# A fused attention and expert kernel: f32 weighted values replaced by three rounded passes, the row of maxima copied by DMA, weight splits moved into the first block

## The reference

```python
q_bits = (np.einsum('bhsd,dk->bhsk', q, proj) > 0).astype(np.int64)
k_bits = (np.einsum('bhsd,dk->bhsk', k, proj) > 0).astype(np.int64)
mask = q_bucket[:, :, :, None] == k_bucket[:, :, None, :]
scores = np.where(mask, scale * np.matmul(q, k.transpose(0, 1, 3, 2)), -1000000000.0)
attn = np.exp(scores - np.max(scores, axis=-1, keepdims=True))
attn = attn / (np.sum(attn, axis=-1, keepdims=True) + 1e-09)
x = np.matmul(attn, v)                      # heads side by side: 1536 x 512
h = x @ w_in                                # 512 x 2048
g = np.where(h > 0.0, h, np.exp(np.minimum(h, 0.0)) - 1.0)
x = g @ w_out                               # 2048 x 512
# rows with x @ w_skip > 0 get x + gate * (relu(x @ w1[e]) @ w2[e]), e = argmax(x @ w_gate)
```

## Time and profile before

| | us |
|---|---|
| median of three runs | 715.51 |
| the profiled execution: time | 718.39 |
| the profiled execution: span from first to last instruction | 716.5 |
| PE busy (matmuls) | 678.6 (95%) |
| DVE, ACT, POOL busy | 326.7, 238.2, 192.9 |

### The profile page before, as it was taken

How to read it: one execution, slowest core, us unless ns; L and a number is a source line. 1 busy time by engine, 2 the same in 40 slices (tenths; PEclk the granted TensorE clock), 3 DMA queues, 4 the chain that set the end, 5 groups by cost and what they waited for, 6 DMA issues and landing times.

```text
span 716.5 us, 9192 instructions
## 1 busy us (share of the span) xinstructions
PE 678.6 (95%) x3472; PEld 574.7 (80%) x3472; DVE 326.7 (46%) x475; ACT 238.2 (33%) x365; POOL 192.9 (27%) x179
## 2 busy tenths in 40 slices
PE   4999999998999999999999999999998975999996
PEld 3677767676777777799999989989997954989995
DVE  6766656565666654133232223222314257446542
ACT  1233334333333334333342334233422321334330
POOL 3322253535162430659120002000002034112111
PEclk9999999999999999999999999999999995999999
DMA  7456656564555530412020002000366765699200
GB/s 176 118 129 141 165 125 163 125 162 96 139 117 133 116 89 10 131 44 67 1 90 1 1 0 88 0 0 0 146 200 206 241 238 188 237 346 334 89 11 24
DMA packets 69235, 83.95 MB, mean 117 GB/s; under 512 B 35540, under 2 KB 45780, under 8 KB 69200
## 3 DMA queue, kind: packets, MB, share of 16 engines
q1 hardware_dynamic: 67920, 79.83, 38.1%
q0 software_dynamic: 1280, 3.65, 1.6%
HBM read 56.64 MB, written 8.44 MB: 91 GB/s over the span
## 4 chain that ended last, share of the span: by engine, by line
PE 85%; DMA 5%; DVE 4%; SPq 2%; ACT 1%; issue 1%; POOL 0%; POOLq 0%; DVEq 0%; ACTq 0%
PE banks L1179 18%; PE banks L1166 18%; PE banks L1125 15%; PE banks L1290 8%; PE banks L1305 6%; PE banks L1093 5%; DMA k_hi_lo_T<-qk_lo_T 4%; PE banks L1112 4%; PE banks L1113 4%; SPq L312 2%; PE banks L1077 2%; PE banks L1197 1%; DVE g_lo L839 1%; PE banks L1101 1%; DVE row_max L770 1%
## 5 line engine op out<-in xcount | busy, mean ns | idle before, releaser
L1125 PE MATMUL banks<-probs,v_ones 128*128 128x384 f32 x384 | 152.8, 490 | 0.3 <-ACT o_and_den L629 0.3
L1166 PE MATMUL banks<-x_hi,w_split 128*128 (+1 forms) x512 | 142.4, 339 | 0.8 <-DVE g L860 0.8
L1179 PE MATMUL banks<-w_split,g_hi 128*128 128x512 f32 x384 | 122.2, 399 | 4.8 <-DVE g_lo L839 4.8
L860 DVE SCALAR_TENSOR_TENSOR g<-exp_min_h,banks 128x384 f32<-128x384 f32 x64 | 35.5, 554 | 198.0 <-ACT exp_min_h L672 197.8
L645 ACT ACTIVATE probs<-banks 128x768 f32<-128x768 f32 x96 | 77.8, 811 | 132.3 <-PE banks L1113 132.3
L770 DVE TENSOR_REDUCE row_max<-banks 128x1 f32<-128x768 f32 x96 | 91.4, 957 | 66.5 <-PE banks L1093 64.7
L1166 PEld LDWEIGHTS banks<-x_hi,w_split 128*128 128x128 f32 x512 | 94.2, 189 | 4.0 <-DVE g L860 1.1
L669 ACT ACTIVATE exp_min_h<-banks 128x384 f32<-128x384 f32 x64 | 31.5, 492 | 181.5 <-PE banks L1166 181.5
L1166 PE MATMUL banks<-x_lo,w_split 128*128 (+1 forms) x256 | 86.3, 337 | 0.0
L1179 PEld LDWEIGHTS banks<-w_split,g_hi 128*128 128x128 f32 x384 | 71.3, 190 | 18.0 <-DVE g_lo L839 6.0
L1093 PE MATMUL banks<-k_hi_rows_T,q_hi_rows_T 96*128 96x384 f32 x192 | 76.8, 487 | 7.8 <-DMA k_hi_lo_T<-qk_lo_T 7.5
(11 more groups left out here) (155 smaller groups left out, 835.0 us busy)
## 6 DMA issues: line engine op xcount, KB each, us to landing
expert_w<-in_moe_w SPq DMA_DIRECT2D x32, 1024.0 KB, 5.3
w_raw<-in_moe_w_in SPq DMA_DIRECT2D x16, 256.0 KB, 3.5
w_raw<-in_moe_w_out SPq DMA_DIRECT2D x16, 256.0 KB, 3.7
qk_nat<-in_q SPq DMA_DIRECT2D x16, 192.0 KB, 4.1
qk_nat<-in_k SPq DMA_DIRECT2D x16, 192.0 KB, 4.3
v_nat<-in_v SPq DMA_DIRECT2D x16, 192.0 KB, 3.0
q_hi_rows_T<-qk_hi_T SPq DMA_DIRECT2D x16, 192.0 KB, 2.7
k_hi_rows_T<-qk_hi_T SPq DMA_DIRECT2D x16, 192.0 KB, 3.0
```

The source lines that it names most:

```text
L860: dve.scalar_tensor_tensor(gb[:, j % 2, :], e_neg[:, j % 2, :], -1.0, banks[:, j % 2, 0:BN], ALU.add, ALU.max).then_inc(s_["g_ready"], 1)
L1125: mm = pe.matmul(banks[:, 6 + b, 0:HALF], v_ones[h % 2][:, s, :], probs[:, n % 4, b * HALF:b * HALF + HALF], start=(s == 0), stop=(s == QT ...
L1166: mm = pe.matmul(banks[:, j % 2, 0:BN], w, x, start=(c == 0 and w is hi and x is x_hi), stop=(c == KC - 1 and w is lo))
L1179: mm = pe.matmul(banks[:, 2 + t, :], g, W[:, j, part, :], start=(j == 0 and i == 0), stop=(j == FT - 1 and i == 2))
```

## The change

- `weighted` makes three passes in float32r (high by high, low by high, high by low; L1211 to L1213 of the changed kernel) in place of one f32 matmul, and follows its step by four steps in place of two. `p_hi` is made by ACT (`high_probs`), `p_lo` by DVE for the steps 1 and 2 of a head and by POOL for the other four (`low_probs`). V is split by ACT (`high_of_v`) and POOL (`low_of_v`); nothing of V's mean is left, so `VSUM`, `mean_of_v`, `centre_v` and the addition in `normalise` go.
- Two extra columns of ones in `p_hi` give the sum that the 1e-9 of the denominator needs; ACT adds it in `outputs`.
- The maxima are one row: DVE writes six partitions of 128 and a DMA on SP brings them to the query row (`copy_minus_maxima`), between the copies of the high rows and of the low rows.
- `T`, `MAX_T` and `BITS` stand earlier or later in the steps; SP's other loads stand ahead of the row copies.
- Four weights are split in attention, at every second head, and twelve in the first block, by ACT (`high_of_w`) and DVE (`low_of_w`). The last three weighted units stand in the first block. x is split in smaller pieces.
- Expert 0's weight is split by POOL in pieces of 512 columns, its second half behind the first gather.

```diff
-EARLY = 9
+EARLY = 4
+LAG = 4
+RING = 4
+WIDE = HALF + 2
+ON_DVE = (1, 2)
...
     a, b = h + 1, h + 2
-    plan = [[], [("MAX", a, 0), ("MAX", a, 1)], [("MAX", a, 2), ("MAX", a, 3)],
-            [("MAX", a, 4), ("MAX", a, 5), ("T", b, 0)], [("VSUM", b, 0), ("MAX_T", a, 0)], [("BITS", b, 0)]][s]
+    plan = [[[], [("MAX", a, 0)], [("MAX", a, 1)]], [[], [("MAX", a, 2)], [("MAX", a, 3)]],
+            [[], [("MAX", a, 4)], [("MAX", a, 5), ("T", b, 0)]], [[], [], [("MAX_T", a, 0)]],
+            [[("BITS", b, 0)], [], []], [[], [], []]][s]
...
+            def copy_minus_maxima(h):
+                sp.wait_ge(s_["neg_done"], h + 1)
+                sp.dma_start(qb[h % 3][NEG_ROW:NEG_ROW + 1, :].bitcast(F32), neg[0:QT, h % 2, :].bitcast(F32))\
+                    .then_inc(s_["neg_copied"], 16)
...
             for h in range(HEADS):
+                if h + 3 < HEADS:
+                    load_qk(h + 3)
+                if h + 2 < HEADS:
+                    load_v(h + 2)
                 if h % 2 and h >= 3:
                     store_rden(h // 2 - 1)
-                if h + 3 < HEADS:
-                    load_qk(h + 3)
+                    if h // 2 <= EARLY:
+                        load_w(h // 2 - 1)
+                    load_rden(h // 2 - 1)
+                if h + 2 < HEADS:
+                    copy_rows(h + 2)
                 if h + 1 < HEADS:
-                    load_mean(h + 1)
-                if 0 < h < EARLY:
-                    load_w(h)
-                if h % 2 and h >= 3:
-                    load_rden(h // 2 - 1)
+                    copy_minus_maxima(h + 1)
+                if h + 2 < HEADS:
+                    copy_low_rows(h + 2)
                 if h % 2 == 0 and h:
                     load_den(h // 2 - 1)
-                if h + 3 < HEADS:
-                    load_v(h + 3)
-                if h + 2 < HEADS:
-                    copy_rows(h + 2)
...
+            def low_probs(n):
+
+                pool.wait_ge(s_["p_hi_ready"], n + 1)
+                if n >= RING:
+                    pool.wait_ge(s_["pv_done"], n - RING + 1)
+                pool.tensor_tensor(p_lo[:, n % RING, :, 0:HALF], probs[:, n % RING, :].rearrange("p (b n) -> p b n", b=2),
+                                   p_hi[:, n % RING, :, 0:HALF].bitcast(F32), ALU.subtract)\
+                    .then_inc(s_["p_lo_pool"], 1)
...
             for h in range(HEADS):
+                if h:
+                    low_probs(QT * h - 2)
+                    low_probs(QT * h - 1)
+                low_probs(QT * h)
+                if h % 2 == 0 and h >= 4:
+                    normalise(h // 2 - 2, *low_ready(QT * h))
+                if h % 2 and h >= 3 and h // 2 <= EARLY:
+                    split_w(h // 2 - 1)
+                if h in (11, 13):
+                    split_x(0, ((h - 11) // 2,))
+                low_probs(QT * h + 3)
                 if 0 < h < HEADS - 1:
-                    centre_v(h + 1)
-                if h < EARLY:
-                    split_w(h)
-                if h % 2 and h >= 3:
-                    normalise(h // 2 - 1)
-                if h in (10, 11):
-                    split_x(h - 10)
+                    low_of_v(h + 1)
...
+            def split_first(g):
+
+                for j in range(HALF_W2):
+                    high, w = w2_hi[:, g, j, :], w2_sb[:, 0, g * HALF_W2 + j, :]
+                    pool.tensor_scalar(high, w, 1.0, 1.0, ALU.mult, ALU.mult).then_inc(s_["w_first"], 1)
+                    pool.wait_ge(s_["w_first"], g * HALF_W2 + j + 1)
+                    low = pool.tensor_tensor(w2_lo[0][:, g * HALF_W2 + j, :], w, high.bitcast(F32), ALU.subtract)
+                low.then_inc(s_["w_lo_ready"], 1)
+
             pool.wait_ge(e_loaded[0], 64)
-            for g in range(2):
-                if g:
-                    pool.wait_ge(s_["h_done"], FT * BLOCKS)
...
+            split_first(0)
...
             for e in range(EXPERTS):
+                if e == 1:
+                    split_first(1)
                 pool.indirect_dma_start(out=xg[:, e, :], out_offset=None, in_=y_rows[:, :],
...
-                    if s == 4 and h + 2 < HEADS:
+                    n = QT * h + s
+                    if s == 3 and h + 2 < HEADS:
                         round_qk(h + 2)
...
+                    exponential(n)
+                    if n:
+                        high_probs(n - 1)
+                    if s == 3 and h:
                         outputs(h - 1)
...
+                    if s == 5 and 0 < h < HEADS - 1:
+                        high_of_v(h + 1)
...
+                    if first and j == 2:
+                        outputs(HEADS - 1)
+                    if first and EARLY <= j + 2 < FT:
+                        high_of_w(j + 2)
...
                 if s == 0:
-                    pe.wait_ge(s_["neg_done"], h + 1)
+                    pe.wait_ge(s_["neg_copied"], 16 * (h + 1))
...
-                mm = pe.matmul(banks[:, 6 + b, 0:HALF], v_ones[h % 2][:, s, :], probs[:, n % 4, b * HALF:b * HALF + HALF],
-                               start=(s == 0), stop=(s == QT - 1))
+                width = HALF if b else WIDE
+                high, low = (x[:, n % RING, b, 0:width] for x in (p_hi, p_lo))
+                to = banks[:, 6 + b, 0:width]
+                pe.matmul(to, v_hi[h % 2][:, t, :], high, start=(t == 0), stop=False)
+                pe.matmul(to, v_hi[h % 2][:, t, :], low, start=False, stop=False)
+                mm = pe.matmul(to, v_lo[h % 2][:, t, :], high, start=False, stop=(t == QT - 1))
```

More of the change, by code:

```diff
@@ L224, in build @@
         rows_copied = [sem(f"rows_copied{i}") for i in range(3)]
-        mean_loaded = [sem(f"mean_loaded{i}") for i in range(HEADS)]
         w_loaded = [sem(f"w_loaded{i}") for i in range(4)]
@@ L253, in consumed, with low_ready @@
             return s_[signal], count
+        def low_ready(n):
+            h, t = n // QT, n % QT
+            if t in ON_DVE:
+                return s_["p_lo_dve"], len(ON_DVE) * h + ON_DVE.index(t) + 1
+            others = [x for x in range(QT) if x not in ON_DVE]
+            return s_["p_lo_pool"], len(others) * h + others.index(t) + 1
         lg_flat = logits[:, :, :].rearrange("p t e -> p (t e)")
@@ L507, in normalise, with split_x @@
                         .then_inc(s_["xt_step"], 1)
[L508 to L509 removed]
                 pool.wait_ge(s_["xt_step"], 2 * pair + 2)
[L511 to L514 removed]
+                pool.sem_inc(s_["xt_ready"], 1)
+            def split_x(n, parts=(0, 1)):
                 pool.wait_ge(s_["xt_ready"], PAIRS // B * (n // 2 + 1))
[L517 to L525 removed]
@@ new lines, in split_x @@
+                for i in parts:
+                    x = XT[:, n // 2 * KC + 2 * i:n // 2 * KC + 2 * i + 2, part]
+                    high = xh[:, 1 - n % 2, 2 * i:2 * i + 2, :]
+                    pool.tensor_scalar(high, x, 1.0, 1.0, ALU.mult, ALU.mult).then_inc(s_["x_step"], 1)
+                    pool.wait_ge(s_["x_step"], 2 * n + i + 1)
+                    for c in range(2):
+                        at = (n // 2 * KC + 2 * i + c) * S + n % 2 * HALF
+                        low = pool.tensor_tensor(x_lo[:, at:at + BN], x[:, c, :], high[:, c, :].bitcast(F32), ALU.subtract)
+                    if i:
+                        low.then_inc(s_["x_ready"], 1)
@@ L861, in block_body @@
                                              ALU.add, ALU.max).then_inc(s_["g_ready"], 1)
+                    if first and j == 1:
+                        dve.wait_ge(s_["pv_done"], QT * HEADS)
                     if j:
@@ L865, in block_body @@
                         g_low(n - 1, FT - 1)
+                    if first and EARLY <= j + 2 < FT:
+                        low_of_w(j + 2)
+                    if first and j == 4:
+                        inverse_den(PAIRS - 1)
                     if not first:
@@ L1138, in _ @@
             for n in range(QT * HEADS):
-                h, s = n // QT, n % QT
-                scores(h, s)
-                units = head_units(h, s)
-                if n >= 2:
-                    weighted((n - 2) // QT, (n - 2) % QT, 0)
-                for unit in units[:1]:
-                    prepare(*unit)
-                if n >= 2:
-                    weighted((n - 2) // QT, (n - 2) % QT, 1)
-                for unit in units[1:]:
-                    prepare(*unit)
-            for s in (QT - 2, QT - 1):
-                for b in range(2):
-                    weighted(HEADS - 1, s, b)
+                scores(n // QT, n % QT)
+                for i, units in enumerate(head_units(n // QT, n % QT)):
+                    for unit in units:
+                        prepare(*unit)
+                    if n >= LAG and i < 2:
+                        weighted(n - LAG, i)
+            weighted(QT * HEADS - LAG, 0)
+            weighted(QT * HEADS - LAG, 1)
+            pe.wait_ge(s_["exp_done"], QT * HEADS)
             pe.wait_ge(s_["gates_loaded"], 32)
@@ L1208, in block_body @@
                     if first:
```

(4 more changed lines are left out.)

255 lines of the change are left out of this document (126 added, 129 removed).

## The result

The changed kernel takes 749.25 us, the median of four runs (747.21 to 750.88), beside 715.19 for the kernel before: a ratio of 1.045, interval 1.038 to 1.053. The forecast was 691 and the range ended at 707. It is wrong in sign. The profiled execution has a span of 747.8 and a time of 749.8.

A forecast was written before the change was run, and what follows sets the result against it. PE's work was taken to set the pace, then the chain of copies at 15.6 us a head. Terms 3.9 - 13.6 - 6.95 - 3.6 - 4.3 + 0.5 = -24.0 gave 691.5, called 691; range 670 to 707.

The forecast's parts named there:

- the last copy's landing: Attention, low-row copies to the next head: last copy lands 3.9 us after issue, the middle value of the earlier trace.
- First result: Head 0, paced by DVE's six maxima and the waits for copies: its result comes at 49.05 instead of 45.15, +3.9 us.
- thirteen results: Attention, results after the first: 5 x 16.8 + 4 x 16.0 + 2 x 16.2 + 2 x 15.6 = 211.6, was 225.2: -13.6 us.
- to expert 0's first product: After head 13's result: -6.95 us up to the last weighted pass, -3.6 in block 3, -4.3 at the blocks' end.
- The rival of late landings: Attention: last low-row copy lands after 7.2 us in every head, heads 18.9, kernel slower at 725; chance 0.04.
- The copied row: Attention: minus maxima, issued at 11.4 behind the copies, land near 15.2, before the next head's scores at 15.5.
- PE's work: Attention, per head: 14.41 us of PE work instead of 16.56, with rounded weighted passes at 0.175 each.
- Step 4's wait for DVE: Attention, each head: step 4's scores wait 0.9 us for DVE's low rows, inside the 1.1 already counted.
- The chain as the pace of a head: Attention: transposes, copies and next head's first maximum take 15.5 us, with slack about 15.6 a head, above PE's work.
- The lock in the even heads: Attention: DVE's subtraction waits 1.7 us for POOL's normalising, making five even heads 16.8 us instead of 15.6.
- First block's splits at nothing: First block: twelve weight splits by ACT and DVE, two steps ahead, hidden by PE: 0; at most 1 us each.
- End of the blocks: Block 3 and blocks' end: shorter POOL holds save 3.6 and 4.3 us; later gathers cost +0.5, between 0 and +2.

The follow-up runs named there:

- the edit alone: Kernel before with only expert 0's second weight split by POOL in 512-column pieces, second half behind the first gather: 711.01 us beside 718.82, ratio 0.991.

## Why the prediction was wrong, step by step

The forecast failed at one step: the last copy's landing, taken at 3.9 us as in the old order of SP. Behind the load on two engines the row of maxima lands after 12.0 us, and six heads become 10.3 us longer. The forecast's terms stand here beside the changed kernel and beside the version with the load cut by rows, all from profiled executions against the one of before. "First result" is its copy-out; the third line is from head 13's result to expert 0's first product, the fourth from there to the end of the span.

| term | forecast | changed | load cut by rows |
|---|---|---|---|
| first result | +3.9 | +7.3 | +6.5 |
| thirteen results | -13.6 | +32.3 | -22.6 |
| to expert 0's first product | -14.9 | -7.0 | -14.3 |
| the rest | +0.5 | -1.3 | -0.6 |
| sum | -24.1 (called -24.0) | +31.3 | -31.0 |

- **The landing of the copies, the step that failed.** "8.0 + 4.04 + 0.64 + 3.9 + 0.14" took 3.9 for the last copy from the earlier trace rows, and "SP's other loads stand ahead of the row copies" was counted as SP's time only. The landing depends on what is queued ahead, and one of those loads keeps two of 16 engines. Behind it the row of maxima lands after 12.02 us, past the worst of 7.2 that the slower rival knew. Of the 3.3 that the 7.2 of the earlier trace rows had above 3.9, 1.9 were that load's doing already; the prediction put them down to weight loads ("those heads had a weight load behind the copies"). With the load cut by rows in the kernel before, and all weight loads in place, the waits are gone and the worst landing is 5.3.
- **The rival of late landings** had the right sign and place, at 0.04. It had them in every head and at 7.2; they are in six of the thirteen and at 12. It also missed the price behind the wait: PE at half clock for 4 us, 2 us each time.
- **The copied row** was said to land "near 15.2" before the scores at 15.5. That holds without the broadcast load (1.7 us of waits in all).
- **PE's work** was nearly right: weighted passes start 0.177 apart. Step 4's wait for DVE was 0.6 on average (8.3 in 14) where 0.9 was taken.
- **The chain as the pace of a head** isn't there once the load is out of the way. The prediction had a head at 15.6 because the next head's first maximum waits for the last copy. In the version with the load cut by rows that wait is 1.1 us in three times, as low rows land after 3.2 in the middle for 3.9; a head of 15.23 is PE's passes (14.41 by the prediction's sum) and the small waits, DVE's above all. That the thirteen heads of that version average 15.6 is luck.
- **The lock in the even heads** (+1.2 in each of five) isn't there. In the version with the load cut by rows the timeline of POOL and DVE has

```profile
125.52 4.48 POOL L539 TENSOR_TENSOR attn_T<-o_and_den,rden_rows 64x768 f32<-64x768 f32 x2
```

```profile
127.33 0.95 DVE L872 TENSOR_TENSOR probs_lo<-probs,probs_hi 128x768 fp32r<-128x768 f32 x1
128.20 0.94 DVE L829 TENSOR_TENSOR qk_lo_T<-banks,qk_hi_T 128x768 fp32r<-128x768 f32 x1
129.26 1.56 DVE L872 TENSOR_TENSOR probs_lo<-probs,probs_hi 128x768 fp32r<-128x768 f32 x1
```

  By the 1.82 of the earlier trace rows POOL's first operation ends at about 127.33. DVE's subtraction starts there and isn't held, and POOL's pair takes 4.48 for 3.64; that DVE got in between the two is read from these times. The low part of q and k runs beside POOL at its full speed, 0.94, as the forecast had it. Only the second subtraction is held, by 0.6, and nothing waits for it. The terms for the lock, 5 x 1.2, 4 x 0.4 and 2 x 0.6, are 8.8 of the 9.0 us by which the forecast's thirteen results, 211.6, lie above the 202.6 of that version; as the 15.6 beneath them was luck, so is how well this fits.
- **First block's splits at nothing.** ACT and DVE were hidden, as said; the load in front of them wasn't, for the same reason as above: 4.1 of waiting and 2 of slow passes.
- **End of the blocks** was right: -7.9 forecast, with +0.5 for the gathers; the edit alone gave 7.6 less in that stretch, and 6 less in time.
- **First result** came 3.4 later than forecast in the changed kernel, and 2.6 later with the load cut by rows. The PE timeline shows about where: the first scores start at 24.62, but until 31.9 the 24 passes of scores and maxima stand 0.32 apart, at half speed, where the kernel before has 0.175 from 25.35 on: some 3.5 us (the stage table gives a granted clock of 1.00 from 25 to 30 us for both and doesn't show it). Why PE is slow there wasn't tested; the mean matmuls, which kept PE at work just before 25.35, are gone.

With the load cut by rows the time, 687.3, lies 4 us from the forecast of 691; there a first result that came too late and a lock that cost nothing cancel in part. What stays open is the share of the 16 us that the order of the units brings, beside the passes.

## What to carry to other kernels

Look at the DMA's busy share beside its GB/s: a stretch at a share of 0.1 with transfers outstanding was here a DMA on two engines of 16. Its cost was not its own landing but that of what was issued behind it within its time, and no wait of PE named it. Before SP's order is changed, list for every DMA that moves what will be queued behind it; write a broadcast with a large dimension outermost (here 64 in place of 2), and take landing times from rows with the same neighbours ahead, not from the median of the old order.

## What was unexpected of the hardware

- A load of 384 KB with outermost extent 2 held a share of 0.1 for some 5 us by itself, landed 11.9 us after its issue in the kernel before and 14.4 in the changed one, and made a 3 KB DMA issued 4.7 us behind it land after 12.02 us. Two of 192 KB with extent 2 did the same; two with extent 64 landed in 3.7 (kernel before) or 3.8 (changed kernel) in the middle. Of the 96 semaphore steps of the six row copies behind it twelve came late, two in 16, and 84 did not.
- While POOL split a weight, small DVE operations on SBUF went from 0.18 to 1.13 (a cast) and from 0.48 to 1.41 (two operands). The Trainium skill, "SBUF — State Buffer", "Who interferes with whom", lists casts among the operations that can be held, though a cast reads one operand; the row of the cast agrees. The forecast's short form of it, that an operation with one SBUF operand stays out, is too wide.
